# When the sums of x and the last rows of y are split into two parts

## The chip, the cores and the metric

One NeuronCore of a Trainium2 chip runs the program. The metric is the device time of one execution in microseconds (us). The program is written engine by engine, with semaphores: TensorE (PE), VectorE (DVE), ScalarE (ACT), GpSimd (POOL), and SyncE (SP), which issues most DMAs. Each engine works strictly through its own list.

## The reference

Three stages follow each other on 3072 tokens (4 sequences of 768) with 384 features:

```python
# attention, per (batch, head), D = 48
cur = u[None] * kt (x) vt
y[:, :, t] = rt . (state + cur)
state = wt[:, :, :, None] * state + kt (x) vt
# first MLP
x = ((y @ w1) * (y @ w2)) @ w3 @ w_out
# mixture of 8 experts; P from 8 rounds of row and column scaling of exp(x @ w_gate)
for e in range(E):
    h = np.maximum(x @ w1[e], 0.0)
    out += P[:, e:e + 1] * (h @ w2[e])
```

All of it is float32. The large products are made of three products of shorter numbers: every operand is kept as a high part (rounded, by ACT) and a low part (the number less its high part, by DVE), and PE adds high by high, high by low and low by high. So each operand needs one ACT and one DVE instruction before PE may use it.

## The kernel before, in words

**Attention and first MLP (0 to about 550 us).** The work goes in 12 units of 256 tokens, each in 8 steps. In step k of unit u PE makes the score level k-1 (`score`; `diag` in step 0), DVE scales R and K for the next level (`level`, lines 1117 and 1119), and ACT copies the scaled R into a padded tile (`pad`, line 812, two copies). PE waits for both before the next level (line 1453; level 5 has its own line, 1447). Beside this, step by step, PE makes one slice up (`go_up`) and one slice down (`go_down`) of the first MLP for units further back; for it ACT copies `a` and rounds `ab`, and DVE multiplies `ab` (line 1167) and makes its low part.

Three smaller things of the units matter here. `make_ruk` (DVE, line 1094) multiplies K and R of the next unit for `diag`; it is made in two halves, one in step 3, one in step 5. `make_y` (PE, step 3, lines 1492 and 1494) makes y of the unit before; ACT copies its last part (`copy_last_y`) and the rest (`copy_y`) as high parts, and DVE makes the low parts (`split_last_y`, `take_x`), both in step 4. POOL copies R of the next unit into the padded tile (`begin_rpad`, line 625) as soon as y's products are done.

**The experts (about 550 us to the end).** The tokens go in three passes of 1024 (`NST`), each in two halves of 512. The 64 slices of all experts' hidden features go in 22 groups per pass (`NG`): first a small group of one slice (`G % NG == 0`, `multiply_first`, 6 products), then 21 full groups of three slices. A full group multiplies 3 slices by 3 blocks of features for 2 halves of tokens in 15 products in place of 18, which need sums of weights and sums of x (`xs`). The 15 are worked through in the order S1, Q5, S2, Q0, S3, Q1, S4, R1, S5, R2, S6, R3, S7, R4, S8; they alternate between two banks of PSUM, so product p may start only when product p-2 has been added up. In each such step DVE adds the product to its block (`add_product`, lines 1265 to 1269), scales finished blocks by the routing weight (`scale`, line 1306) and makes the low part of h (`split_h`, line 1274); ACT copies some products (`copy_product`) and makes the high part of h (`take_h`, line 1009). Between the products PE puts the down projections of earlier blocks (`project_to`). At the start of each pass DVE also takes out the six y of the pass before (`take_y`, lines 1288 and 1290).

The 15 sums of x are made anew for every pass: POOL adds (`sum_x`, lines 735 and 738), ACT rounds (`take_xs`, line 926), DVE makes the low part (`split_xs`, lines 1082 and 1182). A sum takes the place of the one of the pass before as soon as that product of the last full group is done. `x_no` counts the low parts in the order of `x_order`; `multiply_first` and the first full group wait for these counts. The order on DVE and ACT is written out in loops over (G, p): a step's additions first, the sums of x at its end:

```python
if g == NG - 1 and st + 1 < NST and p >= 3:
    split_xs(st + 1, p - 3)
```

In the same way the small group makes the last three at its steps 0 to 2, so that twelve of the fifteen low parts fall into the last full group of a pass and three into the small group after it.

## Time and profile before

| | us |
|---|---|
| median of 3 runs | 2080.27 |
| the three runs | 2076.05 to 2084.07 |
| the profiled execution, its own time | 2073.27 |
| its span, first to last instruction | 2071.4 |
| PE busy in the span | 2012.6 |
| DVE busy in the span | 1357.8 |

The span is one execution as the profiler saw it. A waits view adds up, per line, how long an engine stood idle and which work ended the wait; "issue" means that the profile names no releaser. A timeline view has one row per instruction: start, duration, engine, line, operation, and in brackets the idle time before it. The end of a matmul is modelled, so that of PE the starts are the firm numbers.

### The profile page before, as it was taken

The page shows a single profiled execution, that of the slowest core. Times are in us where ns is not written, and L with a number is a line of the kernel's source. Part 1 is how long each engine was busy: PE and PEld are TensorE (multiplying, and loading weights), DVE is VectorE, ACT ScalarE, POOL GpSimd, SP SyncE. Part 2 cuts the span into 40 slices and gives each one's busy share as a digit, 9 for nine tenths or more (in the row PEclk, how much of TensorE's full clock was granted, in tenths as well). Part 3 has the DMA queues.
Part 4 walks back from the last instruction along what each step waited for, and adds up shares of the span by engine and source line. Part 5 has one row for each costly group of instructions (what it writes and reads, how often), then busy time and mean ns, then how long its engine had stood idle before and what let it go on. Part 6 is the DMA issues. An engine that isn't in the chain of part 4 may idle for free.

```text
span 2071.4 us, 40274 instructions
## 1 busy us (share of the span) xinstructions
PE 2012.6 (97%) x16048; PEld 1672.6 (81%) x16048; DVE 1357.8 (66%) x2129; ACT 790.9 (38%) x1448; POOL 614.1 (30%) x879
## 2 busy tenths in 40 slices
PE   6899999999999999999989999999999999999999
PEld 4699999999777777787868888888877888888887
DVE  3677777783686777777676556655676665566556
ACT  4555554553433333333433333332333333333332
POOL 2466776760565666762030000000020000000000
PEclk9999999999999999999999999999999999999999
DMA  8443343330366676775433444343443445443442
GB/s 214 108 122 98 114 130 99 109 104 18 101 229 224 222 248 241 250 256 200 170 122 132 171 146 161 122 167 136 155 140 113 150 140 175 138 160 132 152 137 97
DMA packets 118585, 316.11 MB, mean 153 GB/s; under 512 B 11920, under 2 KB 45616, under 8 KB 118400
## 3 DMA queue, kind: packets, MB, share of 16 engines
q1 hardware_dynamic: 102768, 259.38, 38.7%
q0 software_dynamic: 14944, 53.68, 7.5%
q8 instruction: 128, 2.10, 0.4%
q10 hardware_dynamic: 688, 0.48, 0.1%
q14 instruction: 57, 0.47, 0.1%
HBM read 239.87 MB, written 71.27 MB: 150 GB/s over the span
## 4 chain that ended last, share of the span: by engine, by line
PE 84%; DVE 8%; issue 3%; ACT 2%; DMA 1%; SPq 0%; POOL 0%; DVEq 0%; ACTq 0%
PE ps L1576 22%; PE ps L1578 22%; PE ps L1577 21%; PE ps L1380 4%; PE ps L1381 3%; PE ps L1382 3%; PE ps L1453 2%; PE ps L1403 2%; DVE tb L1306 1%; DVE xs_lo L1082 1%; PE ps L1492 1%; PE ps L1494 1%; DVE tb L1269 1%; DVE R L1117 1%; ACT h_hi L1009 1%
## 5 line engine op out<-in xcount | busy, mean ns | idle before, releaser
L1009 ACT ACTIVATE h_hi<-tb 128x512 fp32r<-128x512 f32 x378 | 239.0, 632 | 651.4 <-DVE tb L1306 619.8
L1576 PE MATMUL ps<-h_hi,w 128*128 128x512 f32 x1152 | 454.7, 395 | 4.2 <-DVE h_lo L1274 4.0
L1578 PE MATMUL ps<-h_hi,w 128*128 128x512 f32 x1152 | 455.3, 395 | 0.0
L1577 PE MATMUL ps<-h_lo,w 128*128 128x512 f32 x1152 | 454.0, 394 | 0.0
L812 ACT ACTIVATE tb<-ps 128x512 f32<-128x512 f32 x378 | 224.8, 595 | 332.2 <-PE ps L1578 325.9
L1274 DVE SCALAR_TENSOR_TENSOR h_lo<-tb,h_hi 128x512 fp32r<-128x512 f32 x382 | 281.3, 736 | 98.6 <-ACT h_hi L1009 79.6
L1265 DVE TENSOR_TENSOR tb<-tb,ps 128x512 f32<-128x512 f32 x252 | 172.1, 683 | 227.7 <-PE ps L1578 227.3
L1269 DVE TENSOR_TENSOR tb<-ps,tb 128x512 f32<-128x512 f32 x252 | 172.8, 686 | 148.1 <-PE ps L1578 148.1
L1306 DVE SCALAR_TENSOR_TENSOR tb<-tb,Pb 128x512 f32<-128x512 f32 x348 | 253.8, 729 | 18.1
L1576 PEld LDWEIGHTS ps<-h_hi,w 128*128 128x128 f32 x1152 | 216.2, 188 | 57.6 <-issue 7.6
L1577 PEld LDWEIGHTS ps<-h_lo,w 128*128 128x128 f32 x1152 | 217.3, 189 | 50.6
L1578 PEld LDWEIGHTS ps<-h_hi,w 128*128 128x128 f32 x1152 | 216.2, 188 | 49.5
L1576 PE MATMUL ps<-xs_hi,early 128*128 128x512 f32 x504 | 201.3, 399 | 5.7 <-DVE tb L1265 3.0
L738 POOL TENSOR_TENSOR xs_sum<-x 128x512 f32<-128x512 f32 x21 | 34.6, 1660 | 559.3 <-PE ps L1578 559.1
L1578 PE MATMUL ps<-xs_hi,early 128*128 128x512 f32 x504 | 200.0, 397 | 0.0
L1577 PE MATMUL ps<-xs_lo,early 128*128 128x512 f32 x504 | 198.4, 394 | 0.0
L1576 PE MATMUL ps<-xs_hi,late 128*128 128x512 f32 x441 | 174.5, 396 | 8.8 <-DVE tb L1269 5.8
L1578 PE MATMUL ps<-xs_hi,late 128*128 128x512 f32 x441 | 173.2, 393 | 0.0
L1577 PE MATMUL ps<-xs_lo,late 128*128 128x512 f32 x441 | 172.8, 392 | 0.0
L812 ACT ACTIVATE Rpad<-R 64x512 f32<-64x512 f32 (+1 forms) x170 | 110.6, 650 | 162.4 <-DVE R L1117 155.1
L1380 PE MATMUL ps<-x,wab_hi 128*128 128x256 f32 x576 | 171.0, 297 | 1.0 <-DMA x<-yT 1.0
L1382 PE MATMUL ps<-x,wab_lo 128*128 128x256 f32 x576 | 161.8, 281 | 0.0
(159 smaller groups left out, 3299.7 us busy)
## 6 DMA issues: line engine op xcount, KB each, us to landing
early<-w_rows SPq DMA_DIRECT2D x63, 1024.0 KB, 5.5
late<-w_rows SPq DMA_DIRECT2D x63, 896.0 KB, 5.2
w<-w_rows SPq DMA_DIRECT2D x128, 384.0 KB, 4.3
w_rows<-batch POOLq DMA_DIRECT2D x105, 384.0 KB, 3.6
w_rows<-w SPq DMA_DIRECT2D x64, 384.0 KB, 2.7
Pb<-p_rows SPq DMA_DIRECT2D x24, 512.0 KB, 6.0
w_raw<-w POOLq DMA_DIRECT2D x16, 576.0 KB, 6.0
w_raw<-w SPq DMA_DIRECT2D x16, 576.0 KB, 4.7
```

The source lines that it names most:

```text
L812: return nc.scalar.activation(dst, src, ACT.Copy)
L1009: nc.scalar.activation(h_hi[:, slot_of(G, b), :], tb[:, t_of(G, b), :], ACT.Relu).then_inc(h_hi_made, 1)
L1265: ve.tensor_tensor(t, t, bank, ALU.subtract).then_inc(added, 1)
L1269: ve.tensor_tensor(t, bank, t, ALU.add).then_inc(added, 1)
L1274: ve.scalar_tensor_tensor(out=h_lo[:, slot, :], in0=what, scalar=0.0, in1=h_hi[:, slot, :].bitcast(f32), op0=ALU.max, op1=ALU.subtract).th ...
L1306: ve.scalar_tensor_tensor(out=t, in0=what, scalar=0.0, in1=Pb[k % 2][:, 1 - b % 2, :], op0=ALU.max, op1=ALU.mult).then_inc(scaled, 1)
L1380: mm(o, w_hi, x_hi, start=start, stop=False, skip_group_check=shared)
L1381: mm(o, w_hi, x_lo, start=False, stop=False, skip_group_check=shared)
L1382: return mm(o, w_lo, x_hi, start=False, stop=stop, skip_group_check=shared)
L1576: mm(o, w_hi, x_hi, start=start, stop=False, skip_group_check=True)
L1577: mm(o, w_hi, x_lo, start=False, stop=False, skip_group_check=True)
L1578: return mm(o, w_lo, x_hi, start=False, stop=stop, skip_group_check=True)
```

## The change

It has two parts. The first concerns the passes: the fifteen sums of x of a next pass are no longer rounded and split in the old order. They go in three groups, in the last full group, in the small group and in the first full group of the next pass, after a table that says at which product's step each is made. The second concerns the units: both halves of `make_ruk` stand in step 3, and so does `split_last_y`, which no longer waits for the copy of the rest of y; in exchange `copy_y` waits for `split_last_y`, and `take_x` for `copy_y`.

```diff
-        x_order = lambda st: X_FIRST if st == 0 else list(range(NP))
+        X_LOW = [{Q0: S1, R1: Q0, S6: Q1, R3: S5}, {1: R3, 3: S8, 5: Q5},
+                 {S1: S2, S2: S3, Q0: S4, Q1: R1, R1: R2, S5: S6, S6: S7, R3: R4}]
+        X_HIGH = [{S2: S1, S4: Q0, S5: Q1, S6: S5}, {0: R3, 1: S8, 5: Q5},
+                  {S1: S2, Q5: S3, S2: S4, S3: R1, Q1: R2, S4: S6, S5: S7, S6: R4}]
+        X_NEXT = [p for stage in X_LOW for p in stage.values()]
...
+        x_stage = lambda G: (G + 1) % NG if 0 < (G + 1) // NG < NST and (G + 1) % NG < 3 else None
+        x_order = lambda st: X_NEXT if st else X_FIRST
-        x_summed_in = lambda st: [p for p in x_order(st) if p not in X_OWN and p != S3]
+        x_summed_in = lambda st: [p for p in (range(NP) if st else X_FIRST) if p not in X_OWN and p != S3]
...
             def copy_y(u):
                 act.wait_ge(y_made, 2 * u + 2)
+                act.wait_ge(y_split, u + 1)
...
                 if g == 0:
                     if st:
-                        for p in (R4, S8):
-                            take_xs(st, p)
+                        take_xs(st, X_HIGH[1][0])
                         take_h(G - 1, S8)
+                        take_xs(st, X_HIGH[1][1])
                     take_first_h(G, 0)
...
+                    if st:
+                        take_xs(st, X_HIGH[1][5])
                     take_first_h(G, 1)
...
-                    if g == NG - 1 and st + 1 < NST:
-                        if p >= 2:
-                            take_xs(st + 1, p - 2)
+                    if x_stage(G) is not None and p in X_HIGH[x_stage(G)]:
+                        take_xs((G + 1) // NG, X_HIGH[x_stage(G)][p])
...
             def split_last_y(u):
                 dve.wait_ge(y_copied, u + 1)
-                dve.wait_ge(x_copied, u + 1)
...
             def take_x(u):
                 x = x01[u % 2]
+                dve.wait_ge(x_copied, u + 1)
...
-                if 1 <= u <= U and k == 4:
-                    split_last_y(u - 1)
...
-                if u + 1 < U and k in (3, 5):
-                    make_ruk(u + 1, k // 5)
+                if u + 1 < U and k == 3:
+                    make_ruk(u + 1, 0)
+                    make_ruk(u + 1, 1)
+                if 1 <= u <= U and k == 3:
+                    split_last_y(u - 1)
...
-                        if st and p < 3:
-                            split_xs(st, S7 + p)
...
-                    if g == NG - 1 and st + 1 < NST and p >= 3:
-                        split_xs(st + 1, p - 3)
+                    if x_stage(G) is not None and p in X_LOW[x_stage(G)]:
+                        split_xs((G + 1) // NG, X_LOW[x_stage(G)][p])
```

The lists of PE, POOL and SP are the same as before, instruction for instruction and wait for wait. How DVE's list moves is shown at three places. A row has the line in the kernel (some ten lines further down in the changed one), the operation, out<-in, the shape and what it waits for.

**DVE, steps 3 to 5 of a unit.** Before, from the first half of the products K*R (`ruk`) to the second (`yT` is the last part of y, `x_74` the rest of it, `decay` belongs to `level`):

```order
L1094 TENSOR_TENSOR ruk<-K_75,R_77 128x512 [waits diag_made,update_made,r_loaded0,k_loaded0]
L1117 TENSOR_TENSOR R_78<-R_78,decay_83 128x64x8 [waits near_done,decayed,scored]
L1119 TENSOR_TENSOR K_76<-K_76,decay_83 128x64x8
L1122 COPY_PREDICATED near_64<-left_sb,ps 128x32x8
L1127 TENSOR_TENSOR decay_84<-decay_83 128x64
L1167 TENSOR_TENSOR ab<-ps,ab 128x256 [waits a_copied]
L1082 TENSOR_TENSOR yT<-ps,yT 128x256 [waits x_copied,y_copied]
L1082 TENSOR_TENSOR ab_lo<-ab,ab_hi 128x256 [waits ab_hi_made]
L1082 TENSOR_TENSOR x_74<-ps,x_74 128x768
```

and with the change:

```order
L1105 TENSOR_TENSOR ruk<-K_75,R_77 128x512 [waits diag_made,update_made,r_loaded0,k_loaded0]
L1105 TENSOR_TENSOR ruk<-K_75,R_77 128x512
L1093 TENSOR_TENSOR yT<-ps,yT 128x256 [waits y_copied]
L1128 TENSOR_TENSOR R_78<-R_78,decay_83 128x64x8 [waits near_done,decayed,scored]
L1130 TENSOR_TENSOR K_76<-K_76,decay_83 128x64x8
L1133 COPY_PREDICATED near_64<-left_sb,ps 128x32x8
L1138 TENSOR_TENSOR decay_84<-decay_83 128x64
L1178 TENSOR_TENSOR ab<-ps,ab 128x256 [waits a_copied]
L1093 TENSOR_TENSOR ab_lo<-ab,ab_hi 128x256 [waits ab_hi_made]
L1093 TENSOR_TENSOR x_74<-ps,x_74 128x768 [waits x_copied]
```

The second `ruk`, which stood seven rows further down, and the low part of `yT` now stand ahead of the level's scaling of R and K.

**DVE, last full group of the second pass, from the addition of S4.** Before (`xs_lo` are the sums' low parts):

```order
L1269 TENSOR_TENSOR tb<-ps,tb 128x512 [waits copied,multiplied]
L1306 SCALAR_TENSOR_TENSOR tb<-tb,Pb_137 128x512 [waits added,p_loaded1]
L1082 TENSOR_TENSOR xs_lo<-xs_sum,xs_hi 128x512 [waits xs_hi_made]
L1274 SCALAR_TENSOR_TENSOR h_lo<-tb,h_hi 128x512 [waits h_hi_made]
L1182 SCALAR_TENSOR_TENSOR xs_lo<-xw,xs_hi 128x512 [waits xs_hi_made]
L1269 TENSOR_TENSOR tb<-ps,tb 128x512 [waits added,multiplied]
L1306 SCALAR_TENSOR_TENSOR tb<-tb,Pb_137 128x512 [waits added,p_loaded1]
L1082 TENSOR_TENSOR xs_lo<-xs_sum,xs_hi 128x512 [waits xs_hi_made]
L1269 TENSOR_TENSOR tb<-ps,tb 128x512 [waits added,multiplied]
```

and with the change:

```order
L1281 TENSOR_TENSOR tb<-ps,tb 128x512 [waits copied,multiplied]
L1318 SCALAR_TENSOR_TENSOR tb<-tb,Pb_137 128x512 [waits added,p_loaded1]
L1286 SCALAR_TENSOR_TENSOR h_lo<-tb,h_hi 128x512 [waits h_hi_made]
L1093 TENSOR_TENSOR xs_lo<-xs_sum,xs_hi 128x512 [waits xs_hi_made]
L1281 TENSOR_TENSOR tb<-ps,tb 128x512 [waits added,multiplied]
L1318 SCALAR_TENSOR_TENSOR tb<-tb,Pb_137 128x512 [waits added,p_loaded1]
L1281 TENSOR_TENSOR tb<-ps,tb 128x512 [waits added,multiplied]
```

Of three low parts of sums in this stretch one is left; in the whole group four of twelve.

**DVE, first full group of the third pass, from the low part of the block that S4 ends.** Before:

```order
L1274 SCALAR_TENSOR_TENSOR h_lo<-tb,h_hi 128x512 [waits h_hi_made]
L1269 TENSOR_TENSOR tb<-ps,tb 128x512 [waits added,multiplied]
L1306 SCALAR_TENSOR_TENSOR tb<-tb,Pb_130 128x512 [waits added,p_loaded0]
L1269 TENSOR_TENSOR tb<-ps,tb 128x512 [waits added,multiplied]
L1274 SCALAR_TENSOR_TENSOR h_lo<-tb,h_hi 128x512 [waits h_hi_made]
L1306 SCALAR_TENSOR_TENSOR tb<-tb,Pb_130 128x512 [waits added,p_loaded0]
L1269 TENSOR_TENSOR tb<-ps,tb 128x512 [waits copied,multiplied]
L1274 SCALAR_TENSOR_TENSOR h_lo<-tb,h_hi 128x512 [waits h_hi_made]
L1265 TENSOR_TENSOR tb<-tb,ps 128x512 [waits copied,multiplied]
```

and with the change:

```order
L1286 SCALAR_TENSOR_TENSOR h_lo<-tb,h_hi 128x512 [waits h_hi_made]
L1093 TENSOR_TENSOR xs_lo<-xs_sum,xs_hi 128x512 [waits xs_hi_made]
L1281 TENSOR_TENSOR tb<-ps,tb 128x512 [waits added,multiplied]
L1318 SCALAR_TENSOR_TENSOR tb<-tb,Pb_130 128x512 [waits added,p_loaded0]
L1093 TENSOR_TENSOR xs_lo<-xs_sum,xs_hi 128x512 [waits xs_hi_made]
L1281 TENSOR_TENSOR tb<-ps,tb 128x512 [waits added,multiplied]
L1286 SCALAR_TENSOR_TENSOR h_lo<-tb,h_hi 128x512 [waits h_hi_made]
L1318 SCALAR_TENSOR_TENSOR tb<-tb,Pb_130 128x512 [waits added,p_loaded0]
L1281 TENSOR_TENSOR tb<-ps,tb 128x512 [waits copied,multiplied]
L1286 SCALAR_TENSOR_TENSOR h_lo<-tb,h_hi 128x512 [waits h_hi_made]
L1193 SCALAR_TENSOR_TENSOR xs_lo<-xs_sum,xs_hi 128x512 [waits xs_hi_made] x2
```

Four of the eight low parts that this group takes over (R2, S6, and S7 with R4) fall into this stretch.

## Rows read from the trace of the kernel before

**Rows 1.** page, part 1: busy time of each engine over the span

```profile
PE 2012.6 (97%) x16048; PEld 1672.6 (81%) x16048; DVE 1357.8 (66%) x2129; ACT 790.9 (38%) x1448; POOL 614.1 (30%) x879
```

**Rows 2.** windows: busy us of PE, PEld, DVE, ACT, POOL; clock, DMA

```profile
1020.00:1090.00 70.00, 63.09 (x267) 49.33 (x266) 55.72 (x81) 27.61 (x49) 20.40 (x13) 1.00 0.40 135
1090.00:1525.00 435.00, 435.00 (x1889) 352.60 (x1888) 258.36 (x396) 139.96 (x234) 0.00 (x0) 1.00 0.44 149
1525.00:1595.00 70.00, 63.73 (x271) 50.17 (x270) 53.58 (x77) 26.23 (x46) 16.90 (x11) 1.00 0.36 121
```

**Rows 3.** waits of PE, 1030 to 1100: total us, times, longest us

```profile
PE ps L1576 <- issue: 2.3, 1, 2.3
PE ps L1576 <- DVE tb L1269: 1.6, 2, 1.2
PE ps L1576 <- DVE h_lo L1274: 1.4, 1, 1.4
```

**Rows 4.** waits of PE, 1530 to 1620

```profile
PE ps L1576 <- issue: 3.0, 1, 3.0
```

**Rows 5.** timeline, second pass's end: start, us, engine, work [idle <-releaser]

```profile
1542.50 1.78 DVE L1082 TENSOR_TENSOR xs_lo<-xs_sum,xs_hi 128x512 fp32r<-128x512 f32 x1
1554.74 1.78 DVE L1082 TENSOR_TENSOR xs_lo<-xs_sum,xs_hi 128x512 fp32r<-128x512 f32 x1
1558.72 0.67 DVE L1265 TENSOR_TENSOR tb<-tb,ps 128x512 f32<-128x512 f32 x1
1559.50 0.47 PE L1576 MATMUL ps<-xs_hi,first_hi 128*128 128x512 f32 x1 [3.01 <-issue]
```

**Rows 6.** line 1082 (low parts, DVE): count, ns min/median/max

```profile
L1082 DVE TENSOR_TENSOR xs_lo<-xs_sum,xs_hi x27: 677/684/1785, 525.3 to 1565.0; 128x512 fp32r<-128x512 f32 x27
L1082 DVE TENSOR_TENSOR yT<-ps,yT x12: 411/414/415, 76.1 to 506.7; 128x256 fp32r<-128x256 f32 x12
```

**Rows 7.** timeline, third pass's first full group, DVE and PE

```profile
1581.76 0.69 DVE L1274 SCALAR_TENSOR_TENSOR h_lo<-tb,h_hi 128x512 fp32r<-128x512 f32 x1
1582.37 0.68 DVE L1269 TENSOR_TENSOR tb<-ps,tb 128x512 f32<-128x512 f32 x1
1586.54 0.69 DVE L1274 SCALAR_TENSOR_TENSOR h_lo<-tb,h_hi 128x512 fp32r<-128x512 f32 x1
1588.58 0.69 DVE L1265 TENSOR_TENSOR tb<-tb,ps 128x512 f32<-128x512 f32 x1 [1.35 <-PE ps L1578]
1582.82 0.39 PE L1576 MATMUL ps<-xs_hi,late 128*128 128x512 f32 x1
1587.68 0.39 PE L1576 MATMUL ps<-xs_hi,late 128*128 128x512 f32 x1
```

**Rows 8.** waits of PE, 0 to 560

```profile
PE ps L1453 <- DVE K L1119: 7.1, 10, 1.6
```

**Rows 9.** timeline, one unit's fifth step and after, DVE, ACT, PE

```profile
203.77 1.09 DVE L1094 TENSOR_TENSOR ruk<-K,R 128x512 f32<-128x512 f32 x1
205.81 1.27 ACT L812 ACTIVATE Rpad<-R 64x512 f32<-64x512 f32 x2 [2.63 <-DVE R L1117]
207.18 1.09 PE L1453 MATMUL ps<-Rpad,K 128*64 128x128 f32 x16 [0.69 <-DVE K L1119]
```

**Rows 10.** timeline, the same unit's third and fourth step

```profile
192.63 0.68 DVE L1094 TENSOR_TENSOR ruk<-K,R 128x512 f32<-128x512 f32 x1
195.04 0.82 DVE L1117 TENSOR_TENSOR R<-R,decay 128x512 f32<-128x512 f32 x1 [1.73 <-PE ps L1453]
193.09 0.81 ACT L812 ACTIVATE x<-ps 128x768 fp32r<-128x768 f32 x1 [0.56 <-PE ps L1494]
195.89 1.27 ACT L812 ACTIVATE Rpad<-R 64x512 f32<-64x512 f32 x2 [1.99 <-DVE R L1117]
193.19 2.13 POOL L625 COPY Rpad<-R 64x1024 f32<-64x1024 f32 x2 [2.68 <-PE ps L1494]
198.30 0.76 PE L1453 MATMUL ps<-Rpad,K 128*32 128x32 f32 x64
```

More of the change, by code:

```diff
@@ L312, in build_program @@
         X_FIRST = [S1, S5, R3, Q1, Q0, S8, Q5, S2, S3, S4, R1, R2, S6, S7, R4]
-        x_order = lambda st: X_FIRST if st == 0 else list(range(NP))
+        X_LOW = [{Q0: S1, R1: Q0, S6: Q1, R3: S5}, {1: R3, 3: S8, 5: Q5},
[3 more added lines that the diff above has]
+        X_NEXT = [p for stage in X_LOW for p in stage.values()]
+        assert sorted(X_NEXT) == list(range(NP)) and X_NEXT == [p for stage in X_HIGH for p in stage.values()]
+        x_stage = lambda G: (G + 1) % NG if 0 < (G + 1) // NG < NST and (G + 1) % NG < 3 else None
+        x_order = lambda st: X_NEXT if st else X_FIRST
         x_no = lambda st, p: NP * st + x_order(st).index(p) + 1
-        x_summed_in = lambda st: [p for p in x_order(st) if p not in X_OWN and p != S3]
+        x_summed_in = lambda st: [p for p in (range(NP) if st else X_FIRST) if p not in X_OWN and p != S3]
         x_sum_no = lambda st, p: (NP - 4) * st + x_summed_in(st).index(p) + 1
```

## The prediction

> **What bounds the kernel now.** I read the page first. TensorE is busy 97% of the span and VectorE 66% [rows 1], so only time in which TensorE really stands still can be won, and neither part of the change takes work off it. The windows say where it stands still. Between 1090 and 1525, inside the second pass, it is busy for all 435.00 of 435.00. Around the two changes of pass it is busy 63.09 and 63.73 of 70.00 [rows 2]: 6.9 and 6.3 idle, together **13.2 us**. VectorE, by contrast, is busy 55.7 and 53.6 of 70 there against 258 of 435 (59%) inside a pass, and POOL, silent inside the pass, is at work.
>
> The waits name the places. At the first change of pass 1.6 us go in two waits on additions, 2.3 at one wait without a releaser and 1.4 on a low part of h [rows 3]; at the second the wait without a releaser is 3.0 [rows 4]. The timeline gives that one its releaser: DVE's addition of S8 begins at 1558.72 and takes 0.67, so it ends at 1559.39, and PE's first product of the small group begins at 1559.50 [rows 5]. `multiply_first` waits for exactly that addition. DVE is late because the last full group of a pass carries twelve low parts of sums beside its own 21 operations, and some of them run long: 1.78 in two rows [rows 5], where the median is 0.684 [rows 6]. So the cause of the 13.2 us is DVE's queue, not the data.
>
> In the units the waits view shows ten waits of PE on the scaling of R and K, 7.1 us in all, the longest 1.6 in unit 1 [rows 8]; the other nine are (7.1 - 1.6) / 9 = 0.61 each. One of them in full: the second `ruk` starts at 203.77 and takes 1.09, behind it stand R and K, ACT pads from 205.81 for 1.27, to 207.08, and PE starts at 207.18 after 0.69 of standing still [rows 9]. Take `ruk` away and the padding ends a microsecond earlier, before PE is ready at 207.18 - 0.69 = 206.49.
>
> **Part one, the sums of x.** Nothing is added or removed: 15 high and 15 low parts per change of pass, as before. They move from 12 + 3 + 0 (last full group, small group, first full group) to 4 + 3 + 8.
>
> *Won.* Eight low parts leave the last full group. Back to back, operations start 0.60 apart (1581.76 to 1582.37) [rows 7], so 8 x 0.60 = 4.8 us of DVE's queue go, and for those that met POOL up to 1.1 more each (1.785 - 0.677) [rows 6]. The group's waits on additions, the wait for S8's addition and the one for h behind it all come from this queue. All 13.2 us are at stake.
>
> *Left in the last full group.* POOL makes its eleven sums as before, and one low part (of Q0) still stands ahead of S5's addition, with a scaling slowed by POOL behind it. I put down 0.5 per change of pass; between 0 and 1.1, one long operation.
>
> *New in the first full group.* DVE now holds the six y of the old pass (unmoved) and eight low parts. Take the third pass. Today DVE makes a low part of h at 1581.76 and PE starts R2 at 1582.82 [rows 7]. R2's own low part now follows that h: 1581.76 + 0.61 + 0.68 = 1583.05, so PE waits 0.2. From there DVE's queue has been tight up to the low part of h at 1586.54 [rows 7]; the low parts of R2 and S6 now stand in it and S7's right behind it: 1586.54 + 0.60 + 2 x 0.60 + 0.68 = 1589.0, less the some 0.3 that gaps in the queue absorb, 1588.7. PE starts S7 at 1587.68 today [rows 7], so it waits 1.0 in all, R2's 0.2 included. After that DVE has slack again (it idles 1.35 before 1588.58 today [rows 7]). S2, whose high part waits on ACT behind the copy of S1, may cost 0.1. I take 1.2 per change of pass. The bounds: 0, if the gaps absorb more, and 8 x 0.60 - 1.35 = 3.4, if only that one idle stretch takes up the added work.
>
> ACT has the eight high parts in the same group at under a third of its time (139.96 of 435 [rows 2]), hidden. POOL's sum for the pass after next waits for all fifteen low parts, so it now falls behind R4's, with nothing close behind it: free.
>
> Sum of part one: 13.2 - 2 x (0.5 + 1.2) = **9.8 us**; upper end 13.2, lower end 13.2 - 2 x (1.1 + 3.4) = 4.2.
>
> **Part two, the units.** The second `ruk` (1.09 in step 5) goes, which would free the whole wait of 0.61. But it lands in step 3, next to other work. Today DVE makes the first `ruk` there at 192.63, then idles 1.73 until PE's scores let it scale R at 195.04, and POOL copies R into the padded tile from 193.19 for 2.13 [rows 10]. Without POOL the two moved operations take 0.60 + 0.41 (rows of ruk and of yT [rows 6, 10]) and fit into the idle 1.73. With POOL, the second `ruk` (two inputs in SBUF) may lose about a microsecond, as `xs_lo` does (0.68 against 1.785 [rows 6]), while `yT` from PSUM does not (411 to 415 ns in all twelve [rows 6]). Then the scaling of R starts up to 0.8 late.
>
> The added wait sits on ACT: `copy_y` (193.09, 0.81 [rows 10]) now waits for the low part of `yT`, which ends at 192.63 + 0.68 + 0.60 + 0.41 = 194.3, or with POOL in the way about 195.3. Behind it on ACT stands level 3's padding, today 195.89 to 197.16, and PE needs that at 198.30 [rows 10]: a slack of 1.14. So in neither case does PE wait there, but ACT's next copies slip by up to 0.6, and this reaches steps 5 and 6 in place of part of what `ruk` gave. Per unit I get 0.61 at best and 0.3 with POOL in the way; I take 0.45, as the long durations in [rows 6] and [rows 9] say that meeting POOL costs but not always. 9 x 0.45 = 4.1. In unit 1 DVE also makes low parts of weights and the slack is gone before; what it wins at its 1.6 it loses one step earlier: 0, between -1 and +1. The move of `yT` out of step 4 is worth nothing: there it ran in the shadow of ACT's rounding of `ab`. Sum of part two: **4.1 us**, between 1.7 and 6.6.
>
> The Trainium skill, page "SBUF — State Buffer", section "SBUF: two separate sides", has a rule that speaks against this move: VectorE with two SBUF inputs and GpSimd share a port pair that is an exclusive lock, and the one that comes second stands still for the other's whole instruction. The rows on `xs_lo` and `yT` agree with it. By it the second `ruk` always meets POOL's copy, and the sum would be the lower 9 x 0.3 = 2.7 in place of 4.1.
>
> **The sum.** 9.8 + 4.1 = 13.9 us, of which nothing is hidden elsewhere, since PE is what everything else waits for. The profiled execution took 2073.27 and would take 2059.4; it lies 7 us below the median of the runs. Against that median, 2080.27 - 13.9 = **2066.4**. A difference of 0.5%, 10.4 us, is about what a measurement of this kernel can tell from none.
>
> **The rivals.**
>
> *The first full group becomes the bound.* For it: its DVE load rises to 21 + 8 + 6 = 35 operations of 0.60, 21 us, in the time of 33 threefold products of 435.00 / 1889 x 3 = 0.69 each [rows 2], 23 us; every late addition blocks a bank. Against it: today's queue runs dry by 1.35 in its middle. Then part one gives 4.2: 2080.27 - 4.2 - 4.1 = 2072.0. Chance 0.20.
>
> *Part two only trades places.* The moved `ruk` loses to POOL, ACT's copies slip, and the wait of 0.61 stays or moves one score earlier. For it: POOL's copy begins just as the second `ruk` would. Against: the slack of 1.14. Part two gives nothing: 2080.27 - 9.8 = 2070.5. Chance 0.17.
>
> *Slower: step 3 overflows.* If `ruk`, and then R's scaling, each lose to one of POOL's copies, and those stretch in turn, R comes not 0.8 but 1.9 us late, and ACT's padding of level 3 with it. The point from which this decides is the slack of 1.14; beyond it PE waits in step 4, and again for the shifted chain in steps 5 and 6. At 1.9 for 11 units that is 21 us against the 9.8: 2080.27 - 9.8 + 21 = 2091. Against it speaks that POOL's two copies together take only 2.13. Chance 0.05.
>
> **How the numbers follow.** My forecast has 0.58. Its own range is 2061 to 2072; the rival cases at 2070.5 and 2072 lie next to it, and the runs before spread from 4.2 under to 3.8 over their median. The range of 2058 to 2077 leaves out the overflow and the outer tails. Faster by over 0.5%: nearly all of the forecast (0.55), half of the second rival (0.09) and a little of the first (0.03), 0.67. Within: 0.28. Slower: 0.05.
>
> **What would show it.** Right: around the changes of pass PE is busy over 68 of 70; the wait before the small group is gone; a wait of up to 1 us appears at S7 of the second and third pass's first full group; `xs_lo` of 1.78 are rare; the 0.69 waits of the units shrink under 0.3, and the second `ruk` runs over 1 us in step 3. Wrong: waits on additions of 2 us or more in the first full group, or waits on R and K at the step after y.

## The result, and the profile after

| | before | with the change |
|---|---|---|
| median (us) | 2079.93 of 5 runs | 2068.78 of 5 runs |
| the runs | 2076.05 to 2084.07 | 2066.50 to 2070.97 |
| the profiled execution, its span | 2073.27, 2071.4 | 2070.97, 2069.2 |

The ratio is 0.9956 with an interval of 0.994 to 0.9972: the change is faster by 0.44%, which is 9.2 us, between 5.8 and 12.5 (the two medians differ by 11.2). The forecast was 2066.4, with a range of 2061 to 2072. The time is close to it; one of the terms behind it is far off. The forecast also gave 0.67 to "faster by over 0.5%": the measured 0.44% lies just short of that, and its interval reaches to both sides of 0.5%.

The windows of the changed kernel answer to [rows 2]; the columns are busy us of PE, PEld, DVE, ACT and POOL, then the granted clock and DMA.

```profile
1020.00:1090.00 70.00, 65.84 (x271) 50.89 (x270) 57.46 (x81) 27.50 (x49) 18.59 (x13) 0.98 0.41 139
1090.00:1525.00 435.00, 435.00 (x1888) 352.44 (x1888) 258.81 (x396) 139.87 (x234) 0.00 (x0) 1.00 0.44 149
1525.00:1595.00 70.00, 66.09 (x280) 51.47 (x279) 54.55 (x78) 27.04 (x47) 15.87 (x11) 1.00 0.40 134
```

Inside a pass PE is still busy without a break. Around the two changes of pass it now stands still for 4.2 and 3.9 us instead of 6.9 and 6.3; I had forecast under 2. The first window also has a clock below 1.00, which the profiled execution of before had not; this comes back at the end.

The waits of PE from 1500 to 1600 answer to [rows 4], and from 1010 to 1090 to [rows 3] (us in total, times, longest):

```profile
PE ps L1586 <- issue: 1.2, 1, 1.2
PE ps L1586 <- DVE tb L1281: 1.0, 1, 1.0
PE ps L1586 <- DVE xs_lo L1193: 0.7, 1, 0.7
PE ps L1586 <- DVE tb L1277: 0.6, 1, 0.6
PE ps L1586 <- DVE h_lo L1286: 0.2, 1, 0.2
...
PE ps L1586 <- DVE tb L1277: 2.1, 1, 2.1
PE ps L1586 <- DVE tb L1281: 1.0, 1, 1.0
PE ps L1586 <- DVE xs_lo L1193: 0.7, 1, 0.7
PE ps L1586 <- ACT tb L821: 0.2, 1, 0.2
```

The wait in front of the small group was 3.0 and is 1.2. The waits on additions (`tb`) are still there, one of them 2.1. New is the 0.7 on `xs_lo` of line 1193, the low part for S7, in both first full groups.

In the units, the row that answers to [rows 8]:

```profile
PE ps L1457 <- DVE K L1130: 1.5, 1, 1.5
PE ps L1463 <- DVE K L1130: 0.7, 1, 0.7
```

Of ten waits on K at line 1453 (now 1463) one is left. It is unit 1's, which was 1.6 before; the other row is unit 1's wait before its level 5, 1.5 in place of 1.3. The nine of 0.61 are gone.

**Where the time went.** The two profiled executions differ by 2.3 us only, though the medians differ by 11.2. So I cut each into stretches at PE's own starts: from the first product of a group to that of the next, and from y to y in the units. In the profiled execution of the changed kernel the first change of pass has these three starts (the last full group of the first pass, then the first and second full group of the next):

```profile
1029.46 0.39 PE L1586 MATMUL ps<-xs_hi,early 128*128 128x512 f32 x1
...
1066.85 0.40 PE L1586 MATMUL ps<-xs_hi,early 128*128 128x512 f32 x1
...
1091.22 0.46 PE L1586 MATMUL ps<-xs_hi,early 128*128 128x512 f32 x1
```

The last full and the small group together took 1066.85 - 1029.46 = 37.39, the first full group 24.37. The same was done for three profiled executions of before, two of the change and one of each experiment:

```
us                              before (3)         change (2)
eleven units, y to y            429.6 429.9 429.9  424.5 424.4
first pass                      473.5 476.4 474.8  476.9 477.3
last full + small, 1st change   39.76 39.77 39.75  37.39 37.09
first full group, 2nd pass      22.97 22.96 22.96  24.37 24.37
rest of the second pass         439.18 each        439.22 439.22
last full + small, 2nd change   38.89 38.89 39.20  35.51 35.52
first full group, 3rd pass      22.97 22.96 22.96  24.36 24.38
rest of the third pass          439.18 each        439.16 439.17
start to the first y            69.2 72.8 70.8     71.0 70.1
```

A stretch that the edit touches repeats to 0.3 us or better, and the two cases of 0.3 (37.39 and 39.20) have a piece at a lower TensorE clock in them, of which the last section tells. The start, with its loads, and the first pass differ by 3 to 4 us between executions of one and the same kernel. With the change's second execution (e0 below; 37.09, 35.52) against the first of before, the edit moved: units -5.2, the two stretches -2.7 and -3.4, the two first full groups +1.4 each. The sum is -5.24 - 2.67 - 3.37 + 1.40 + 1.41 = **-8.5 us**.

### The profile page after: what moved, and what is told of

Same layout as the page of the kernel before. It is cut to its first block, busy times and chain, and to the rows that moved or that the text cites. A ratio compares the mean times of both kernels' runs of the same rounds, so it can differ in the third digit from the quotient of the medians.

```text
span 2069.2 us, 40264 instructions
## 1 busy us (share of the span) xinstructions
PE 2018.8 (98%) x16048; PEld 1673.5 (81%) x16048; DVE 1359.0 (66%) x2129; ACT 789.0 (38%) x1448; POOL 611.5 (30%) x879
## 4 chain that ended last, share of the span: by engine, by line
PE 86%; DVE 7%; issue 3%; ACT 2%; DMA 1%; SPq 0%; POOL 0%; DVEq 0%; ACTq 0%
PE ps L1586 21%; PE ps L1588 21%; PE ps L1587 21%; PE ps L1390 5%; PE ps L1391 4%; PE ps L1392 4%; PE ps L1463 2%; DVE tb L1318 2%; PE ps L1413 2%; ACT h_hi L1019 1%; DVE xs_lo L1093 1%; PE ps L1502 1%; DVE tb L1281 1%; PE ps L1504 1%; DVE h_lo L1286 1%
## 5 line engine op out<-in xcount | busy, mean ns | idle before, releaser
L1318 DVE SCALAR_TENSOR_TENSOR tb<-tb,Pb 128x512 f32<-128x512 f32 x348 | 255.3, 734 | 18.1
L1390 PE MATMUL ps<-x,wab_hi 128*128 128x256 f32 x576 | 170.8, 297 | 1.5 <-DMA x<-yT 1.5
L1391 PE MATMUL ps<-x,wab_hi 128*128 128x256 f32 x576 | 161.7, 281 | 0.0
```

The source lines that it names most:

```text
L1318: ve.scalar_tensor_tensor(out=t, in0=what, scalar=0.0, in1=Pb[k % 2][:, 1 - b % 2, :], op0=ALU.max, op1=ALU.mult).then_inc(scaled, 1)
L1390: mm(o, w_hi, x_hi, start=start, stop=False, skip_group_check=shared)
L1391: mm(o, w_hi, x_lo, start=False, stop=False, skip_group_check=shared)
```

## The experiments

Each was measured beside runs of before on the same chip. Edits are shown against the changed kernel unless said otherwise, without their small companions; `...` marks what is left out. The theory at the start: DVE's queue in the last full group sets the waits that are left, and eight low parts were too few to take out of it, or the wrong thing to take.

**The parts, one by one.** e0 is the change again, e1 has the sums of x alone, e2 the units alone. In e1:

```diff
...
+                if 1 <= u <= U and k == 4:
+                    split_last_y(u - 1)
...
-                if u + 1 < U and k == 3:
-                    make_ruk(u + 1, 0)
-                    make_ruk(u + 1, 1)
+                if u + 1 < U and k in (3, 5):
+                    make_ruk(u + 1, k // 5)
...
```

> The change itself, once more, as the yardstick of the other runs on the same chip. Both theories: 11 us below the kernel before (between 8 and 14).

> Part one alone (the three groups of sums), the units as before. Theory A (each part is worth what its waits in the profiles lost: 13.0 us of waits around the changes of pass became 7.7): 5 to 6 us below the kernel before, and the nine waits of 0.6 in the units are back. Rival B (the longer first pass of the changed kernel's profile, 3.9 us from the units to the first change of pass, comes with part two): 5 to 6 us below as well, but with the first pass as short as before. Rival C (the forecast's 9.8): 9 to 10 us below.

> Part two alone (both products K*R and y's last low part in step 3), the sums as before. Theory A: 5 to 6 us below the kernel before, since nine waits of 0.61 go and none comes; the waits around the changes of pass stay at 13 us. Rival B: only 1 to 2 us below, because the first pass gets 3.9 us longer with it.

```
                ratio to before         units   stretches     first full groups
e0 change       0.9949 (0.9936-0.9962)  424.4   37.09 35.52   24.37 24.38
e1 sums only    0.9982 (0.9973-0.9992)  429.5   37.09 35.55   24.37 24.36
e2 units only   0.9970 (0.9960-0.9979)  424.3   39.75 38.88   22.97 22.96
```

Each part moves its own stretches and no others. Part one is worth 2.67 + 3.37 - 2.81 = 3.2 us by the stretches and 3.7 (1.7 to 5.6) by the ratio; part two 5.3 and 6.2 (4.4 to 8.3). The parts add up. So part two is the larger one, against the forecast of 9.8 and 4.1. Part one is below the 5 to 6 us that the shrunken waits promised: theory A of e1 had left out what the first full group gives back, 2 x 1.4.

**Which half of part two.** e5 puts y's low part back into step 4 and drops the wait that came with it.

```diff
             def copy_y(u):
                 act.wait_ge(y_made, 2 * u + 2)
-                act.wait_ge(y_split, u + 1)
...
+                if 1 <= u <= U and k == 4:
+                    split_last_y(u - 1)
...
-                if 1 <= u <= U and k == 3:
-                    split_last_y(u - 1)
```

> The change, with y's last low part back in step 4 (its waits as before); both products K*R in step 3. The forecast's claim that moving y's low part is worth nothing: the time of the change to within 1 us, and the eleven units from y to y as short as with the change (424.4 us against 429.6 before). Rival E (it is half of the units' gain): 2 to 3 us above the change.

Measured 0.9954 (0.9939 to 0.9968), units 424.47 against 424.37. The move of `yT` and its new wait are worth nothing; the whole of part two is `ruk`.

**Is it POOL?** In the changed kernel DVE's list in the last full group is shorter than before and PE still waits. The timeline of DVE and POOL there (start, duration):

```profile
1050.56 1.65 DVE L1093 TENSOR_TENSOR w<-w_raw,w 128x384 fp32r<-128x384 f32 x1
1052.13 1.75 DVE L1093 TENSOR_TENSOR xs_lo<-x,xs_hi 128x512 fp32r<-128x512 f32 x1
1053.80 0.67 DVE L1277 TENSOR_TENSOR tb<-tb,ps 128x512 f32<-128x512 f32 x1
...
1050.35 2.98 POOL L747 TENSOR_TENSOR xs_sum<-x 128x512 f32<-128x512 f32 x2 [2.85 <-PE ps L1588]
...
1054.53 0.51 PE L1586 MATMUL ps<-xs_hi,late 128*128 128x512 f32 x1 [2.09 <-DVE tb L1277]
```

While POOL makes two sums, two operations of DVE take 1.65 and 1.75; the addition behind them is late, and PE waits 2.09 for it. Counted over the last full and the small group, nine operations of DVE are so lengthened (over 0.9 us) at each change of pass. Against the 0.68 (0.55 for `w`) that they take alone they lose 5.7 and 5.3 us in before, and 6.4 and 5.3 with the change: the low parts have left, this loss has not.

A rival is that the sums themselves come late. The waits of ACT, which is the first to need them, over the same stretch (1028 to 1067) speak against it:

```profile
ACT h_hi L1019 <- DVE tb L1318: 18.0, 8, 4.6
ACT tb L821 <- PE ps L1588: 3.3, 3, 2.1
ACT h_hi L1029 <- DVE tb L1318: 1.4, 1, 1.4
```

It never waits for POOL, and neither does DVE. The test is e3b. It keeps the lists of all engines but lets POOL add only 32 of the 512 columns; ACT and DVE read a part of x in place of the sum, so the work of PE, ACT and DVE stays the same in shape and number, and only POOL's becomes short. For passes 2 and 3 it thus computes with wrong sums of x.

```diff
-                to = xs_sum[:, p, :]
+                n = 32 if st else TW
+                to = xs_sum[:, p, 0:n]
...
-                    what = xs_sum[:, p, :]
+                    what = x_tile(st, X_SUM.get(p, (1,))[0]) if st else xs_sum[:, p, :]
```

> The change, with most of POOL's sums of x for the second and third pass left out: POOL adds only the first 32 of 512 columns, and ScalarE and VectorE take a part of x itself in the sum's place, with the same number and shape of instructions. Theory A (what waiting is left in the last full groups comes from VectorE's operations that run 1.4 to 1.75 us instead of 0.68 because they meet a POOL sum): the time from the first product of the last full group to that of the next pass's first full group falls from 37.1 and 35.5 us to 33 or less, and the time falls by 4 to 6 us below the change. Rival D (VectorE has too many operations there, POOL or not): the two stretches fall by less than 1.5 us each and the time by less than 2 us.

Measured 0.9915 (0.9894 to 0.9936), the stretches 31.86 and 31.36, the first full groups unchanged at 24.40 and 24.38. The same operations of DVE:

```profile
1046.98 0.55 DVE L1094 TENSOR_TENSOR w<-w_raw,w 128x384 fp32r<-128x384 f32 x1
1047.45 0.74 DVE L1094 TENSOR_TENSOR xs_lo<-x,xs_hi 128x512 fp32r<-128x512 f32 x1
1048.12 0.68 DVE L1278 TENSOR_TENSOR tb<-tb,ps 128x512 f32<-128x512 f32 x1
```

And all the waits of PE from 1000 to 1090:

```profile
PE ps L1587 <- DVE xs_lo L1194: 0.7, 1, 0.7
PE ps L1587 <- issue: 0.3, 1, 0.3
```

None of DVE's operations there is over 0.9 us any more. This settles it. DVE has room for its whole list in the last full group, if POOL keeps quiet; meeting POOL costs PE 37.09 - 31.86 = 5.2 and 35.52 - 31.36 = 4.2 us. The gain is larger than theory A had it: by the median 7.8 us below e5, which was measured beside it and has the change's time, in place of 4 to 6. This is also the shortest change of pass seen in any run: before lost 39.76 - 31.86 = 7.9 and 38.89 - 31.36 = 7.5 against this, 15.4 in all. That is more than the 13.2 of idle time, since here a wait costs more than its idle time: before 1054.53 above PE is counted busy up to the modelled end of its last product (0.39 after the start), though the next could have started 0.23 after it, and from a start after a wait to the next start it takes 0.34 in place of 0.23. Some 0.3 per wait goes in this way.

**The same sums at another time.** A sum may take its old one's place only when that product of the last full group is done. e4 has POOL make S8's sum ahead of those of R1, R2, S6, S7 and R4, so that all six fall behind the group's last product.

```diff
-        x_summed_in = lambda st: [p for p in (range(NP) if st else X_FIRST) if p not in X_OWN and p != S3]
+        x_summed_in = lambda st: [Q5, S2, Q0, Q1, S4, S8, R1, R2, S6, S7, R4] if st else [p for p in X_FIRST if p not in X_OWN and p != S3]
```

> The change, with POOL's sums in the order Q5, S2, Q0, Q1, S4, S8, R1, R2, S6, S7, R4: the five that only the first full group needs are made after the last full group has ended, where VectorE idles in the small group. Theory A: the two stretches of 37.1 and 35.5 us fall by about 3 us each, some of it comes back in the first full group, and the time falls by 2 to 5 us below the change. Rival D: no difference beyond 1 us, or slower, if the small group's low parts now meet POOL and come late.

Measured 0.9937 (0.9923 to 0.9951), the stretches 35.53 and 34.37: 1.6 and 1.2 us off, 2.7 in all, by moving POOL's work alone: half of what theory A had for the stretches. The median is 3.2 us below e5's, measured beside it, inside theory A's 2 to 5. Nothing came back in the first full groups (24.36 and 24.39). POOL now stands idle for 11 us and then adds without a break:

```profile
1049.76 2.97 POOL L747 TENSOR_TENSOR xs_sum<-x 128x512 f32<-128x512 f32 x2 [10.97 <-PE ps L1588]
1052.69 3.44 POOL L744 TENSOR_TENSOR xs_sum<-x 128x512 f32<-128x512 f32 x2
1056.09 3.42 POOL L747 TENSOR_TENSOR xs_sum<-x 128x512 f32<-128x512 f32 x2
...
1049.88 1.72 DVE L1286 SCALAR_TENSOR_TENSOR h_lo<-tb,h_hi 128x512 fp32r<-128x512 f32 x1
1051.52 0.68 DVE L1277 TENSOR_TENSOR tb<-tb,ps 128x512 f32<-128x512 f32 x1
...
1058.31 1.75 DVE L1093 TENSOR_TENSOR xs_lo<-x,xs_hi 128x512 fp32r<-128x512 f32 x1
```

The addition of a product from PSUM (1051.52, 0.68) runs at full speed in the middle of a sum; the operations with both inputs in SBUF do not. The longest wait that is left, 1.3, is on R3's low part, the last row.

**Taking R3's low part out of the small group.** e7 is e4 with it made at S8's step, and S7's at R2's step; e8 has the second of these alone, without e4's order.

```diff
...
-        X_LOW = [{Q0: S1, R1: Q0, S6: Q1, R3: S5}, {1: R3, 3: S8, 5: Q5},
-                 {S1: S2, S2: S3, Q0: S4, Q1: R1, R1: R2, S5: S6, S6: S7, R3: R4}]
-        X_HIGH = [{S2: S1, S4: Q0, S5: Q1, S6: S5}, {0: R3, 1: S8, 5: Q5},
+        X_LOW = [{Q0: S1, R1: Q0, S6: Q1, R3: S5, S8: R3}, {3: S8, 5: Q5},
+                 {S1: S2, S2: S3, Q0: S4, Q1: R1, R1: R2, S5: S6, R2: S7, R3: R4}]
+        X_HIGH = [{S2: S1, S4: Q0, S5: Q1, S6: S5, R4: R3}, {1: S8, 5: Q5},
...
```

> The late sums (e4), and two entries of the table moved: R3's low part, which needs no sum, at the last product's step of the last full group instead of in the small group, where PE waited 1.3 us for it; and S7's low part one step earlier in the first full group, where PE waited 0.7 us for it. Theory A (each of these waits is that one operation's lateness): the stretch over the last full and the small group falls from 35.5 and 34.4 to about 34.3 and 33.2, the first full group from 24.4 to 23.7 to 23.9, and the time by 2.5 to 4 us below e4. Rival D (VectorE is simply full, so a wait only moves on): less than 1 us below e4.

> The change, with S7's low part one step earlier in the first full group (at R2's step, its high part where it was). Forecast's reckoning (PE waits there for this one operation): the first full group falls from 24.37 to 23.6 to 23.9 us, and the 0.7 wait goes. Rival D: it stays within 0.2 of 24.37, since S6's addition is late instead.

e7 is a miss: 0.9967 (0.9955 to 0.9979), the stretches 38.45 and 37.88, 2.9 and 3.5 us longer than e4's, which neither theory had. The timeline says why:

```profile
1557.06 1.70 DVE L1092 TENSOR_TENSOR xs_lo<-x,xs_hi 128x512 fp32r<-128x512 f32 x1 [1.22 <-ACT xs_hi L936]
1558.68 1.75 DVE L1285 SCALAR_TENSOR_TENSOR h_lo<-tb,h_hi 128x512 fp32r<-128x512 f32 x1
...
1560.57 0.77 PE L1585 MATMUL ps<-h_hi,w 128*128 128x512 f32 x1 [3.39 <-DVE h_lo L1285]
```

The low part stood at the head of DVE's queue before ACT had its high part (1.22 idle); it and the low part of h behind it each met a sum, and PE waited 3.39 for h. In all PE stood still 1.6 us longer than in e4 at each change. The remaining 1.3 and 1.9 come with pieces at half clock, of 3.4 and 6.8 us (see the last section). The part about S7 held: first full groups of 24.12 and 23.64, in e8 24.11 and 23.66, and the 0.7 wait gone; in the second pass one of 0.3 before the next group has come in its place. e8's one run took 2068.56, too few to rank.

**Both mended.** e9 is e4 with S7's low part at R2's step. e10 adds R3 again, now its high part at R3's step and its low part at S7's, ahead of POOL's late sums (shown against e9):

```diff
-        X_LOW = [{Q0: S1, R1: Q0, S6: Q1, R3: S5}, {1: R3, 3: S8, 5: Q5},
+        X_LOW = [{Q0: S1, R1: Q0, S6: Q1, R3: S5, S7: R3}, {3: S8, 5: Q5},
-        X_HIGH = [{S2: S1, S4: Q0, S5: Q1, S6: S5}, {0: R3, 1: S8, 5: Q5},
+        X_HIGH = [{S2: S1, S4: Q0, S5: Q1, S6: S5, R3: R3}, {1: S8, 5: Q5},
...
```

> This is e4 (GpSimd's sums in the late order) with S7's low part of x made at R2's step, before R2's own products are wanted. e4 lost 35.5 and 34.4 us in the last full and small group of the two passes and 24.37 in the first full group; e8 had 24.1 and 23.65 for that group alone. If the two edits add: stretches 35.5 and 34.4, first full groups 24.1 and 23.65, so about 1 us below e4 (2064.5). If the early low part meets another sum: first full groups 24.1, last stretches longer than 35.5, and nothing gained.

> This is e9 with R3's high part made at R3's step and its low part at S7's step of the last full group, ahead of GpSimd's late sums. Theory A (the 1.3 us wait in the small group is for R3's low part, made beside a sum): that wait goes, at most 0.5 comes back at S8's addition, the two stretches are about 34.8 and 33.6 instead of 35.5 and 34.4, and the time is 1 to 1.5 us below e9. Theory D (VectorE has no room left in the last full group, a wait taken away only moves): the stretches are no shorter than e9's, or longer, as they were in e7.

```
        median    ratio to before         stretches     first full groups
e4      2065.41   0.9937 (0.9923-0.9951)  35.53 34.37   24.36 24.39
e9      2063.41   0.9913 (0.9899-0.9928)  35.54 34.39   24.09 23.60
e10     2062.97   0.9909 (0.9892-0.9925)  34.18 34.19   24.13 23.62
```

e9's stretches came out as expected: the two edits add. e10 took 1.4 off the first stretch, as theory A has it, and 0.2 off the second, as theory D. The wait on R3's low part went in both, but at the second change of pass the wait before the small group took its place:

```profile
1551.75 1.78 DVE L1285 SCALAR_TENSOR_TENSOR h_lo<-tb,h_hi 128x512 fp32r<-128x512 f32 x1
1553.45 0.68 DVE L1276 TENSOR_TENSOR tb<-tb,ps 128x512 f32<-128x512 f32 x1
...
1554.23 0.47 PE L1585 MATMUL ps<-xs_hi,first_hi 128*128 128x512 f32 x1 [1.23 <-issue]
```

In e9 that wait of 1.2 was there at the first change of pass only. e9 and e10 cannot be told apart by their times. Both beat the changed kernel: their intervals lie wholly below both of its own (0.994 to 0.9972 and 0.9936 to 0.9962), though these were measured on other chips, and the stretches are shorter by 1.6 and 1.1 in e9 and by 2.9 and 1.3 in e10. How much they win is less sure: the stretches and units put e9 12.0 and e10 13.8 us below before, the ratios 18.1 and 18.9, with intervals that begin at 15.0 and 15.6. What makes up the difference was not found.

**The runs of before.** b1 and b2 are the kernel before, profiled twice more.

> The kernel before, once more with a profile. The three profiles with part two have a first pass 3.1 to 3.8 us longer than the two without it (476.6 to 477.3 against 473.5 and 473.8 us from the first product of the first full group to that of the last). Theory A (chance of how POOL's transfers fall): this profile of the kernel before lies anywhere between 473 and 478. Rival B (part two costs it): 473.5 again, within 0.3.

> The kernel before, a third profile: which of its stretches are the same from one execution to the next and which are not. Expected: eleven units 429.6 to 429.9, last full and small group 39.8 and 38.9, first full group 22.97 each time; the start to the first y anywhere from 69 to 73 and the first pass from 473 to 478.

They took 2080.03 and 2076.84. Their stretches stand in the table above: what the edit touches repeats, and the length of the first pass (473.5, 476.4, 474.8) does not. So rival B is refuted as it was put, and e5 and e4, with both `ruk` in step 3 too, have 474.0 and 474.6. A smaller cost is not ruled out: the ten profiles with both `ruk` in step 3 have a mean first pass of 475.9 us, the four without of 474.6, each group spreading by some 3.

## Why the prediction was right, and which steps were not

**What bounds the kernel.** Right. PE standing still at the changes of pass and in the units was what there was to win, and the stretches shrank there, while those within the passes stayed at 439.2.

**Part one: won and left.** This is the step that failed: "I put down 0.5 per change of pass", left in the last full group. The stretches shrank by 2.7 and 3.4, and against e3b 5.2 and 4.2 us were left, against the 0.5 forecast for each and the upper bound of 1.1. That is 6.0 won there in place of 13.2 - 1.0 = 12.2. Part one gave 3.2 us instead of 9.8, below its own lower end of 4.2. I had counted what DVE carries and taken the list as the cause: eight low parts fewer, so the queue runs free. The rows of 1.78 [rows 5] were before me and I priced them for the operations that leave, and for one scaling that stays. What stays (the scalings, the low parts of h and of `w`) meets POOL's sums just the same: nine lengthened operations before, nine after. e3b shows that the list, at its full length in the changed kernel, is not the bound once POOL is quiet; e4 shows that POOL's timing alone is worth 2.7.

The Trainium skill, page "SBUF — State Buffer", section "SBUF: two separate sides", has the exclusive lock from which this follows: of a DVE operation with two SBUF inputs and a GpSimd operation that reads SBUF, the one that starts first has the port pair for its whole instruction, and the other waits. The traces agree in size (0.68 becomes up to 1.79 and 0.55 becomes 1.65 beside sums of 1.3 to 1.7, and 0.68 stays 0.68 with one input in PSUM). I had applied it to the second `ruk`, where it did not matter, and in the last full group to one operation only, where it mattered for nine.

**Part one: the first full group.** Right: 1.2 forecast, 1.4 measured in both, and in the places named. In the changed kernel's third pass:

```profile
1578.80 0.68 DVE L1093 TENSOR_TENSOR xs_lo<-xs_sum,xs_hi 128x512 fp32r<-128x512 f32 x1
1579.54 0.50 PE L1586 MATMUL ps<-xs_hi,late 128*128 128x512 f32 x1
1584.60 1.29 DVE L1193 SCALAR_TENSOR_TENSOR xs_lo<-xs_sum,xs_hi 128x512 fp32r<-128x512 f32 x2
1585.34 0.50 PE L1586 MATMUL ps<-xs_hi,late 128*128 128x512 f32 x1 [0.66 <-DVE xs_lo L1193]
```

R2's product starts 0.28 late, at the end of its low part (forecast 0.2), and S7's 0.83 late (forecast 1.0 together with R2's). Each restart adds 0.11. With the 0.1 that S2 loses (Q0's product behind it starts 0.08 late, forecast 0.1) this makes up the 1.4. POOL makes no sums there, so the forecast of plain queueing held. The rival that this group becomes the bound (4.2 for part one through a loss of up to 3.4 here) fell, though part one did come out even lower, for the other reason.

**Part two.** 4.1 forecast, 5.2 measured, inside the 1.7 to 6.6. The term that was mis-sized is the 0.45 per unit between "0.61 at best and 0.3 with POOL in the way", and for two reasons. The first is that POOL is seldom in the way. The line of `ruk` in the changed kernel (count, ns min/median/max):

```profile
L1105 DVE TENSOR_TENSOR ruk<-K,R x24: 682/684/1527, 8.5 to 425.1; 128x512 f32<-128x512 f32 x24
```

Of the eleven second halves in step 3 only three are long (1.52 to 1.53), at 24.67, 74.58 and 194.41; the other eight take 0.68 to 0.69. Before the three long ones POOL's copy had begun 0.13 to 0.58 us earlier. In five of the other eight it begins 0.01 to 0.16 us later, and there POOL's copy is lengthened, from 1.03 to between 1.42 and 1.57. So what the forecast made of the Trainium skill's rule, that the second `ruk` always meets POOL's copy and loses, is not what happens; that the one that starts first goes on undisturbed fits these rows. The other reason is that in the one of the nine regular units where `ruk` did lose, PE lost nothing. That one is the unit of [rows 9, 10]. With the change:

```profile
193.80 2.13 DVE L1105 TENSOR_TENSOR ruk<-K,R 128x512 f32<-128x512 f32 x2
195.85 0.41 DVE L1093 TENSOR_TENSOR yT<-ps,yT 128x256 fp32r<-128x256 f32 x1
196.19 1.19 DVE L1128 TENSOR_TENSOR R<-R,decay 128x512 f32<-128x512 f32 x1
...
196.35 0.81 ACT L821 ACTIVATE x<-ps 128x768 fp32r<-128x768 f32 x1 [2.65 <-issue]
197.41 1.28 ACT L821 ACTIVATE Rpad<-R 64x512 f32<-64x512 f32 x2 [0.25 <-DVE R L1128]
...
199.39 0.76 PE L1463 MATMUL ps<-Rpad,K 128*32 128x32 f32 x64
...
207.67 1.09 PE L1463 MATMUL ps<-Rpad,K 128*64 128x128 f32 x16
```

The pair of `ruk` takes 2.13 in place of 1.28. `copy_y` on ACT starts at 196.35, right behind the low part of `yT`, which ends at 195.85 + 0.41 = 196.26, and the padding ends at 197.41 + 1.28 = 198.69. PE starts at 199.39 with no wait: of the slack of 1.14, 0.7 is left. By PE's start the unit stands 199.39 - 198.30 = 1.09 later than in before, so R's scaling began only 196.19 - 1.09 - 195.04 = 0.06 late. The forecast's "up to 0.8 late" does not follow from its own terms either, which give 0.60 + 0.41 + 1.0 - 1.73 = 0.3. And the wait at 207 is gone. What ACT loses in step 3 is caught up before step 5, where I had let half of the gain go. Nearly the whole 0.61 came back nine times (5.5, against 5.2 measured); unit 1, put at 0 between -1 and +1, lost 0.2. That the move of `yT` is worth nothing was right. The sum of 2.7, which the forecast had for the case that POOL is always met, was too low: the pair lost 0.85 in one of these nine units, and PE nothing. The rivals "part two only trades places" and "step 3 overflows" fell.

**The sum.** Forecast -13.9; the stretches give -3.2 - 5.3 = -8.5, and the ratios -9.2 in the first comparison (5.8 to 12.5) and -10.6 (7.9 to 13.3) in e0. So 8.5 lies in both intervals, but below both middle values. The other experiments show the same: added up as above, the stretches of e3b give the 17.7 of its ratio, and all others give less than theirs, by 0.4 to 3.3 us, and e9 and e10 by 6.1 and 5.2. What lies in this rest stays open. The start and the first pass are not in the sum, and the clock is a candidate. In 58 executions of before, beside the experiments, the mean granted clock averaged 0.9973 at a mean of 2078.2 us; in the eleven of the change it was 0.9981 at 2067.8. If time at half clock cost half its length everywhere, this difference of 0.0008 would be 1.6 us. But at the changes of pass it cost less than that, as the last section shows, so 1.6 is an upper value and not a measured term.

That the forecast of 2066.4 was met so well is therefore in part luck. By the stretches its sum was too large by 13.9 - 8.5 = 5.4: one term too large by 6.6, the other too small by 1.1. The time shows only 2.4 of this (2068.78 against 2066.4), since the two medians of five executions differ by 11.2 rather than 8.5, and the median that the forecast started from was 0.3 above the later one. Of its signs, the wait of up to 1 us at S7 and the end of the units' waits came out as described. `ruk` of over 1 us in step 3 came in three units of eleven, and `xs_lo` of 1.78 went from two to one per change of pass. Two did not come: PE busy 68 of 70, and no wait before the small group.

## What to carry to other kernels

A list that is too long and a list that is slowed from outside look alike in a waits view; before taking work out of a queue, compare the durations in it with those of the same line elsewhere, and look up what the neighbour engine does in the long ones. Here the neighbour's timing (one line, POOL's order) was worth nearly as much as rearranging fifteen operations of DVE and ACT. And look at every instance: of eleven moved operations three became slower. The one in a regular unit cost nothing, since the slack behind it was larger than what it lost, so price the slack, not the operation. Lastly, cut two profiles at the bound engine's own landmarks: that showed a change of 1.4 us in a kernel whose executions differ by 8.

## What the runs showed of the hardware that was not expected

**Short stretches at half clock.** The clock under 1.00 in the first window of after comes from one stretch:

```profile
1050.00:1055.00 5.00, 2.91 (x13) 1.91 (x12) 4.90 (x6) 0.73 (x2) 2.93 (x2) 1.00 0.20 79
1055.00:1060.00 5.00, 4.95 (x16) 3.45 (x15) 4.20 (x7) 1.79 (x3) 1.28 (x1) 0.66 0.75 236
```

After PE's wait of 2.09 it ran for 3.4 us with its products 0.43 apart in place of 0.23, that is at 1.2 in place of 2.4 GHz, and then at the full level again. I counted such stretches in the fourteen profiled executions, leaving out the very end: 27, of 3.4 us or twice that. Each began within a wait of PE of 2.0 to 3.5 us or less than 2 us after one; no shorter wait stood alone before one. But not every such wait had one behind it: the 3.01 of [rows 5] had none. At the changes of pass there were such stretches in three of eight cases in before and e2, which has its passes, in two of ten in the change, e1, e5 and e8 (e5's 39.24 in place of 37.1 is one of 6.8 us), and in both of e7's, with its waits of 3.4; and in none of the eight in e3b, e4, e9 and e10, whose longest wait there is 1.3. Over many runs the mean granted clock says the same: 0.9971 in e7 (12 runs), 0.9973 in before, 0.9981 in the change, 0.9986 in e4 and e9 (10 runs).

What such a stretch cost depended on the waits behind it. PE's own work takes longer: without its waits the stretch over the last full and the small group is 37.39 - 3.13 = 34.3 us in after, with 3.4 us at half clock in it, and 37.09 - 4.35 = 32.7 in e0, without. But while PE runs slower, the engines that it would wait for catch up: e0's wait of 1.23 before the small group isn't there in after, and the whole differs by 0.3. In b1 the second change has a half-clock stretch (clock 0.66 from 1566 to 1571) and took 38.89, as before did without one; its wait of 1.4 for h is gone. In b2 it was 0.0 and 0.3. The 6.8 us in e5 cost 2.15. So at these places 3.4 us at half clock cost between nothing and 0.3, not 1.7, and a cost of over 1 us is seen only for e5 and, by the subtraction above, for e7, whose waits of 3.4 stand before it. That the change has fewer of these stretches because its waits are shorter is what the numbers suggest; no run varied the length of one wait by itself to show it.

**Both sides slow down.** Where DVE and POOL meet, POOL loses too: its sums take 1.29 alone and 3.44 for two in a row beside DVE, and its copy in the units 1.03 alone and up to 1.57 behind a `ruk`.
